# Row factors turned once as nine columns, sent to DRAM and loaded back over the partitions, in place of nine wide transposes

## The reference, cut to what matters

```python
a = softmax(causal(q @ k.T / 8));  local = a @ v
q_p = phi(q);  mem = (q_p @ M_prev) / (q_p @ z_prev + 1e-6)
out = g * mem + (1 - g) * local        # g = sigmoid(beta) of the head
```

## Time and profile before

| | us |
|---|---|
| median of 3 runs | 1121.03 |
| lowest, highest | 1120.95, 1123.28 |
| the profiled execution's own time | 1122.92 |
| its span in the trace | 1121.1 |
| PE busy | 1076.2 (96%) |
| DVE busy | 677.8 (60%) |
| ACT busy | 298.4 (27%) |
| POOL busy | 192.5 (17%) |

### The profile page before, as it was taken

One profiled execution on the slowest core, in us unless ns is written; L12 is line 12 of the kernel. 1 busy time (PEld: TensorE's weight loads), 2 busy tenths in 40 slices (PEclk: granted clock), 3 DMA queues, 4 the chain that ended last, 5 costly groups with the idle time before them and its releaser, 6 DMA issues.

```text
span 1121.1 us, 16386 instructions
## 1 busy us (share of the span) xinstructions
PE 1076.2 (96%) x6080; PEld 966.3 (86%) x6080; DVE 677.8 (60%) x1278; ACT 298.4 (27%) x737; POOL 192.5 (17%) x202
## 2 busy tenths in 40 slices
PE   5999999999889999999999999899999999999998
PEld 2667676676879999999999999898999999899997
DVE  5676766767388544545454468865656565565654
ACT  3666666666432212112121123301001010000100
POOL 3434434344265000000000025500000000000000
PEclk9999999999889999999999999999999999999999
DMA  4322121220134000000000014100000000000000
GB/s 162 119 97 101 52 101 56 98 101 20 38 113 132 1 1 1 0 0 0 0 0 0 0 37 131 57 1 13 15 0 28 0 28 0 0 28 0 28 0 28
DMA packets 16599, 44.56 MB, mean 40 GB/s; under 512 B 1968, under 2 KB 1968, under 8 KB 16560
## 3 DMA queue, kind: packets, MB, share of 16 engines
q1 hardware_dynamic: 16560, 44.05, 11.3%
HBM read 39.33 MB, written 4.72 MB: 39 GB/s over the span
## 4 chain that ended last, share of the span: by engine, by line
PE 89%; DVE 6%; issue 3%; ACT 1%; DMA 1%; SPq 0%; DVEq 0%
PE ps L473 35%; PE ps L494 18%; PE ps L486 17%; PE ps L450 8%; PE ps L384 3%; DVE pt_lo L751 2%; PE ps L379 1%; PE ps L459 1%; PE ps L428 1%; PE ps L418 1%; PE ps L387 1%; DVE x_all L795 1%; ACT r_rows L570 1%; PE ps L405 1%; DVE h_hi L824 1%
## 5 line engine op out<-in xcount | busy, mean ns | idle before, releaser
L473 PE MATMUL ps<-x_hi,w 128*128 128x384 f32 x1536 | 392.5, 336 | 0.0
L473 PEld LDWEIGHTS ps<-x_hi,w 128*128 128x128 f32 x1536 | 280.9, 189 | 7.4
L473 PE MATMUL ps<-x_lo,w 128*128 128x384 f32 x768 | 258.3, 336 | 0.0
L486 PE MATMUL ps<-h_hi,w 128*128 128x384 f32 x768 | 196.6, 336 | 6.0 <-DVE h_lo L826 6.0
L494 PE MATMUL ps<-w,h_hi 128*128 128x512 f32 x576 | 179.2, 392 | 3.1 <-DVE h_lo L826 3.1
L824 DVE CAST h_hi<-act_tmp 128x384 fp32r<-128x384 f32 x192 | 108.9, 567 | 100.9 <-PE ps L486 53.2
L486 PEld LDWEIGHTS ps<-h_hi,w 128*128 128x128 f32 x768 | 139.5, 189 | 7.0 <-DVE h_lo L826 7.0
L473 PEld LDWEIGHTS ps<-x_lo,w 128*128 128x128 f32 x768 | 144.7, 188 | 0.0
L296 POOL TENSOR_TENSOR w<-stage,w 128x1024 f32 (+1 forms) x32 | 77.7, 2436 | 358.3 <-ACT w L544 358.3
L486 PE MATMUL ps<-h_lo,w 128*128 128x384 f32 x384 | 129.0, 336 | 0.0
L494 PEld LDWEIGHTS ps<-w,h_hi 128*128 128x128 f32 x576 | 106.8, 188 | 22.1 <-issue 2.4
(11 more groups left out here) (110 smaller groups left out, 1233.8 us busy)
## 6 DMA issues: line engine op xcount, KB each, us to landing
nat<-nat_in SPq DMA_DIRECT2D x16, 768.0 KB, 5.4
qk<-qk_t SPq DMA_DIRECT2D x16, 608.0 KB, 3.8
stage<-w_in SPq DMA_DIRECT2D x32, 256.0 KB, 2.7
stage<-w_out SPq DMA_DIRECT2D x32, 256.0 KB, 2.9
out<-rows_out SPq DMA_DIRECT2D x18, 256.0 KB, 2.1
beta_sb<-beta SPq DMA_DIRECT2D x1, 4.0 KB, 6.5
```

Source lines behind the costliest of these rows:

```text
L473: mm = pe.matmul(ps[:, bank:bank + CHUNK], w[:, n, wp, 0, cols], xp[:, m, :], start=(m == 0 and part == 0), stop=(m == KM - 1 and part == 2))
L486: mm = pe.matmul(ps[:, Y_AT + 512 * m:Y_AT + 512 * m + CHUNK], w[:, n, wp, 1, cols], hp[:, n % 2, :], start=(n == 0 and part == 0), stop=( ...
```

## The change

`r_nat` gets its nine columns in the order in which they are sent (three POOL instructions in place of one). A chunk R, between C2 and C3 in slot 3, transposes these nine columns at once into 9 partitions x 128. ACT copies that to `r_turned`. SP writes `r_turned` to the DRAM tensor `r_dram`, waits for its arrival, and issues four loads that read it back with one row repeated over 64 partitions each, into `r_rows`. `store_x` waits for these loads. The RMAIN chunk, the transpose at L436 and the copies at L570, L591 and L592 are gone. `spread_r(g - 1)`, with the write, its wait and the four loads, stands on SP ahead of `load_qk(g + 1)` and `load_nat(g + 1)`. The order of the ring is now G, C00, C01, C10, C11, C2, R, C3, PHI, TAIL.

```diff
-G, C00, C01, C10, C11, C2, C3, RMAIN, PHI, TAIL = range(10)
+G, C00, C01, C10, C11, C2, R, C3, PHI, TAIL = range(10)
-SLOT_CHUNKS = ((G,), (C00, C01), (C10, C11), (C2, C3), (RMAIN, PHI, TAIL))
+SLOT_CHUNKS = ((G,), (C00, C01), (C10, C11), (C2, R, C3), (PHI, TAIL))
@@ sync
+            def spread_r(p):
+                sp.wait_ge(r_done, p + 1)
+                sp.dma_start(r_dram[p % 2], r_turned[0:2 * FULL + 1, :]).then_inc(r_sent, 16)
+                sp.wait_ge(r_sent, 16 * (p + 1))
+                if p >= 1:
+                    sp.wait_ge(x_stored, p)
+                for a in range(2):
+                    main = r_dram[p % 2, FULL * a:FULL * a + FULL].rearrange("i q -> (i q)").rearrange("(o x) -> o x", o=1)
+                    tail = r_dram[p % 2, 2 * FULL:2 * FULL + 1, REST * a:REST * a + REST]
+                    sp.dma_start(r_rows[D * a:D * a + D, 0:EDGE], main.to_broadcast([D, EDGE])).then_inc(r_loaded, 16)
+                    sp.dma_start(r_rows[D * a:D * a + D, EDGE:S], tail.to_broadcast([D, REST])).then_inc(r_loaded, 16)
-            for p in range(1, PAIRS):
-                load_qk(p)
-                load_nat(p)
-                if p == 2:
+            load_qk(1)
+            load_nat(1)
+            for g in range(1, PAIRS + 1):
+                spread_r(g - 1)
+                if g + 1 < PAIRS:
+                    load_qk(g + 1)
+                    load_nat(g + 1)
+                if g == 1:
                     for n in range(STAGES):
@@ tensor, turn
-                elif c == RMAIN:
+                elif c == R:
                     pe.wait_ge(r_ready, p + 1)
-                    for i in range(FULL):
-                        for a, rows in ((1, P), (0, D)):
-                            r = r_nat[:, u, 2 * i + a:2 * i + a + 1].to_broadcast([P, rows])
-                            mm = pe.transpose(ps[0:rows, at + P * i:at + P * i + P], r, ident[:, :])
+                    mm = pe.transpose(ps[0:2 * FULL + 1, at:at + P], r_nat[:, u, 0:2 * FULL + 1], ident[:, :])
...
-                    pe.transpose(ps[:, at:at + P], phi[:, u, LAST, :], ident[:, :])
-                    r = r_nat[:, u, 2 * LAST:2 * LAST + 1].to_broadcast([P, P])
-                    mm = pe.transpose(ps[:, at + P:at + 2 * P], r, ident[:, :])
+                    mm = pe.transpose(ps[:, at:at + P], phi[:, u, LAST, :], ident[:, :])
@@ scalar, round_chunk
-                        act.wait_ge(x_stored, p)
-                    act.activation(r_rows[:, 0:EDGE], ps[:, at:at + EDGE], ACT.Copy).then_inc(r_done, 1)
+                        act.wait_ge(r_sent, 16 * p)
+                    act.activation(r_turned[0:2 * FULL + 1, :], ps[0:2 * FULL + 1, at:at + P], ACT.Copy).then_inc(r_done, 1)
...
-                    act.activation(r_rows[0:D, EDGE:S], ps[0:D, at + P:at + P + REST], ACT.Copy)
-                    act.activation(r_rows[D:P, EDGE:S], ps[D:P, at + P + REST:at + 2 * P], ACT.Copy)
@@ vector, store_x
-                dve.wait_ge(r_done, p + 1)
-                dve.wait_ge(pt_hi_done, LOS * (p + 1))
+                dve.wait_ge(r_loaded, 64 * (p + 1))
```

More of the change, by code:

```diff
@@ L57, in live, with build @@
     return not isinstance(count, int) or count > 0
-def build(nc, qk_t, nat_in, beta, w_in1, w_out1, w_in2, w_out2, out):
+def build(nc, qk_t, nat_in, beta, w_in1, w_out1, w_in2, w_out2, r_dram, out):
     base = (nc.sbuf_base + 31) // 32 * 32
@@ L115, in build @@
     r_rows = sb("r_rows", [S])
+    r_turned = sb("r_turned", [P])
     ident = sb("ident", [P])
@@ L177, in build @@
     r_done = semaphore("r_done")
+    r_sent = semaphore("r_sent")
+    r_loaded = semaphore("r_loaded")
     pv_done = semaphore("pv_done")
@@ L329, in factors @@
                     pool.wait_ge(gate_step, 9)
-                pool.tensor_tensor(r_nat[:, u, :], inv[:, u, 0:2 * QT], rest_by[:, m].rearrange("p i a -> p (i a)"), ALU.mult).then_inc(r_ready, 1)
+                for a in range(2):
+                    r = inv[:, u, 0:2 * FULL].rearrange("p (i a) -> p a i", a=2)[:, a]
+                    rest = rest_by[:, m, 0:FULL, a]
+                    pool.tensor_tensor(r_nat[:, u, FULL * a:FULL * a + FULL], r, rest, ALU.mult)
+                pool.tensor_tensor(r_nat[:, u, 2 * FULL:2 * FULL + 1], inv[:, u, 2 * LAST:2 * LAST + 1], rest_by[:, m, LAST, 0:1], ALU.mult).then_inc(r_ready, 1)
                 pool.tensor_tensor(f_nat[:, u, :], den[:, u, 0:2 * QT], inv[:, u, 2 * QT:4 * QT], ALU.mult).then_inc(f_step, 1)
@@ L390, in chunk_free @@
             def chunk_free(p, c):
-                if c >= 2 and c - 2 == RMAIN:
+                if c >= 2 and c - 2 == R:
                     pe.wait_ge(r_done, p + 1)
@@ L413, in turn @@
                 elif c in (C2, C3):
-                    t = 2 + c - C2
+                    t = 2 if c == C2 else 3
                     for a in range(2):
@@ L566, in round_chunk @@
                 act.wait_ge(turned, CHUNKS_OF * p + c + 1)
-                if c == RMAIN:
+                if c == R:
                     if p >= 1:
-                        act.wait_ge(x_stored, p)
-                    act.activation(r_rows[:, 0:EDGE], ps[:, at:at + EDGE], ACT.Copy).then_inc(r_done, 1)
+                        act.wait_ge(r_sent, 16 * p)
+                    act.activation(r_turned[0:2 * FULL + 1, :], ps[0:2 * FULL + 1, at:at + P], ACT.Copy).then_inc(r_done, 1)
                     return
@@ L908 @@
     out = nc.dram_tensor("out", (TOKENS, DM), F32, kind="ExternalOutput").ap()
-    build(nc, *args, out)
+    r_dram = nc.dram_tensor("r_dram", (2, 2 * FULL + 1, P), F32).ap()
+    build(nc, *args, r_dram, out)
     result = run_bass_kernel_spmd(nc, [arrays], core_ids=[0])
```

## The result

The changed kernel took 1263.95 us (median of 4 runs, 1263.71 to 1267.96) against 1122.03 us (4 runs): a ratio of 1.127, 95% interval 1.125 to 1.130. That is 142 us slower; 129 were forecast, and the time lies inside the range.

What follows compares the result with a forecast made beforehand. PE was taken to bound the kernel. Held loads 94, low clock 35 and PE 0.6 made 130 us on 1122.92, 1252.5; less the 1.9 us median offset, 1251 us. Own range 1225 to 1280; 8 in 10, 1203 to 1300.

Steps and rivals of the forecast that it cites:

- Where the bound lies: Whole kernel: PE, busy 96% of the span and 89% of the chain, sets the end; SP issues every load.
- PE's terms: PE in slots 3 and 4: 1.4 us saved, 0.1 added, about 1.5 idle ahead of C3; net +0.3 us a pair.
- The hold: SP's `qk` and `nat` loads go out behind R's copy and round trip; G starts 6.7 us later, 14 times, 94 us.
- The clock: PE behind G: idle gaps lower the clock to 1.2 GHz in each held pair, 2.5 us each, 35 us.
- The clock holds: Rival, PE at G: scores break the idleness and the clock level stays or is back; 1216 us, chance 0.15.
- Dearer round trip: Rival: write nears 6.5 us, small loads hold `nat`, or low clock reaches slot 2; 1282 to 1313 us, chance 0.12.
- second condition: In the rival with chance 0.12: the small loads of the factors hold up `nat`.
- Loads not held: Rival: `nat` lands before ACT reaches `exp_q`; only +0.3 us in 16 pairs remains, 1126 us, chance 0.03.
- faster: Rival: loads not held and C3's wait absorbed; 1.3 us saved in 16 pairs, 1100 us, chance 0.02.

Runs made afterwards that it cites:

- the first experiment: Changed kernel with the loads of the pair after next and the first weights issued on SP ahead of the factors' spreading: 1124.20 us, ratio 1.0025.
- PE kept busy: Changed kernel with 44 unread transposes behind slot 4 of groups 1 to 14 and 36 zero-adding matmuls behind the next group's first scores: 1229.62 us.
- the loads beside the write: Changed kernel with `qk` and `nat` issued between the write of the factors and the wait for it: 1208.08 us, ratio 1.0779.
- two of the experiments: Changed kernel with next loads ahead of the factors' spreading, 1124.20 us; that order with R turned in C3's bank, no chunk R, 1101.34 us.

## Why the prediction was right

**Where the bound lies.** Right: the change was priced on SP, an engine with no share of the chain before, and the first experiment shows that its place in SP's order was all of the 140 us.

**PE's terms.** Right. 1.4 us saved in slot 4, 1.3 us of idleness ahead of C3 (1.5 forecast), both in the shadow of the hold: +0.2 us a pair where the hold is gone, +0.3 forecast.

**The hold, 6.7 us a pair.** Right in mechanism, 0.6 us too small: 7.3 us. Its steps, from the write on (measured: the mean of the 14 pairs, `nat` landed when `exp_q` starts):

| step | forecast | measured |
|---|---|---|
| write to next issue | 2.15 us | 1.3 us |
| the four loads, to the issue of `qk` | 1.8 us | 2.5 us |
| `qk` to `nat` | 0.44 us | 0.7 us |
| landing of `nat` | 5.4 us | 5.9 us |
| landing of `nat` to G | 2.65 us | 2.7 us |

The steps add up to 13.08 us where 12.44 were forecast. The first four add up to 10.2 us in the pair behind 230.68, and to 11.3 in the one behind 202.18, where one issue took 1.34 us; 9.8 was forecast. The price of the write was taken from a transfer 57 times its size and was 0.9 us too high. The price of an issue, 0.44 us, was taken from the big loads: of the four loads that repeat one row over 64 partitions the first takes 0.45 us to issue and the others 0.6, and `qk` behind them 0.58. These two errors nearly cancel up to the issue of `nat`, 4.5 us behind the write on average where 4.4 were forecast; that this part came out is luck. What remains is the landing: I named the 0.9 us by which the small loads could delay `nat` and counted them as nothing, and 0.5 came. Whether the small loads caused it is not shown.

**The clock, 2.5 us a pair.** Right in mechanism, 0.3 us too small: 2.8 us, from G to the next write (14.5 us, against 11.7 with the loads first and 11.7 in twelve of the 14 pairs with PE kept busy). The low level stood behind G in every held pair, where G's four transposes took 1.11 or 1.12 us, and it lasted to about 6 us behind G, though PE had worked on the scores before. So of the two counts in the prediction, 3.1 us if the time counts from G and 1.2 if it counts from the scores, the first was nearly right. The Trainium skill, "TensorE: Matmul & The Clock Gate", section "HAM oscillation — how this bites in real kernels", which the prediction cites, tells of a loop that starts each tile cold; the trace agrees, with 0.50 behind G in every held pair. But not every wait for a DMA has this effect: with the loads beside the write one pair kept 1.00.

Together the two terms explain the miss: 0.6 + 0.3 us in 14 pairs are the 13 us between 129 and 142.

**The rivals.** "The clock holds" would have been 1216; the added work on PE made it hold in twelve of 14 pairs, and that run took 1230; the rest is the hold, about 1 us a pair longer there than the 6.7 forecast. "Dearer round trip" fell as far as the round trip goes: from the write to the issue of `qk` the changed kernel took 3.8 us, and 3.95 were forecast. Only its second condition, a later `nat`, came about, by half a microsecond. "Loads not held" and "faster" fell for the kernel as changed, and they are what two of the experiments built: 1124 us (1126 forecast for that case) and 1101 us (1100 forecast).

The things to be seen in the profile were there: a period of 27.6 us (forecast 26.7; forecasts in brackets from here on), `nat` issued 4.35 us behind the write in the pair at 230.68 (4.4), ACT waiting 7.7 us on average (9), PE idle 3.5 to 5.2 us ahead of the scores (3.7). Only the wait ahead of G was shorter, 1.6 us against 2 to 3, because the scores in between ran at half speed and filled it.

## What to carry to other kernels

A queue that issues in order has a critical place even where it has no critical work: before a wait is added to it, look at what is issued behind that wait and how much spare time it has. Here five small DMAs with two waits cost 10 us a pair ahead of the loads and next to nothing behind them, and most of that was there as soon as the loads stood behind the first of the two waits. The price is not the idle time alone: 2.8 of the 10 us were PE's lower clock behind its gaps. And a chunk put into a ring of two buffers changes what its neighbours wait for; a free corner of a buffer that is turned anyway cost no wait here.

## What the hardware showed that was not expected

- A write of 4.5 KB from SBUF to DRAM released SP's next issue 1.2 us after its own start, in nearly all of the 16 pairs; rows of 256 KB to `out` take 2.0 to 2.1 us.
- How long an issue holds SP's queue depends on what was issued just before it. Of four loads in a row that repeat one DRAM row over 64 partitions, the first took 0.45 us and the others 0.60 us, whether the row has 2 KB or 256 bytes. The same load of `qk` (608 KB over 128 partitions) took 0.58 us behind these four and 0.34 us ahead of them. Single issues took up to 1.37 us in the changed kernel. Why is open.
- An idle stretch of 2.39 us ahead of one instruction was followed by the low level in the kernel before; one of 2.54 us, with the loads beside the write, was not. Behind one of 3.19 us in that run G's four transposes still ran at the upper level (0.66 us), and the clock fell only after them, within 236 to 238. The length of one gap alone does not tell whether the clock falls.
